# A delta-rule scan with two expert layers: the masked product of q and k with q's transposes narrowed first

## The chip, the cores and the metric

The kernel runs on one core of a Trainium2 chip. The metric is the device time of one launch in microseconds (us). Three runs of the kernel before took 901.98, 902.17 and 902.83 us, so the median is 902.17.

## The reference

Three parts follow each other; the change is in the first.

```python
# part 1: B, H, S, D = 4, 8, 768, 48
k_n = k / (norm(k) + 1e-6)
for t in range(S):
    y[t]  = q[t] @ state
    state = state + beta[t] * outer(k_n[t], v[t] - state.T @ k_n[t])
# part 2: x is y as (3072, 384)
h = x @ w_in; x = maximum(0.01 * h, h) @ w_out          # 2048 hidden
# part 3: 8 experts, routed per row
do = (x @ w_skip) > 0; e = argmax(x @ w_gate)
out = x + do * p[e] * (maximum(x @ w1[e], 0) @ w2[e])
```

## The kernel before

**Number form.** Nearly every matmul operand is held as two float16 parts, HI and LO. A product is three matmuls (HI·HI, LO·HI, HI·LO), the list `PARTS`. The HI part is a copy by ScalarE (`*_high`, all at L954), the LO part a subtraction by GpSimd or VectorE.

**Part 1 in groups.** The 768 steps are cut into 12 groups g of 64 (C). There are 32 heads in all; two of them lie on the 128 partitions, so a group has 16 units u (NU), in four steps of four (PAIRS). The scan needs, for each unit, the 64x64 products of a group's keys with its keys (`gram_a`) and of its keys with its queries (`gram_p`), the second masked to the entries above the diagonal.

- `turn_k`, `turn_q` (SyncE's queue) transpose the keys and queries of a group by DMA into `kT` and `qT`. Both are 128x128 per unit with two diagonal 64x64 blocks; the rest is zero.
- `compact_k` copies kT's two diagonal blocks by DMA next to each other into `kTc`, which is 64 columns wide.
- `gram_a(g, st)` is 12 matmuls of 64 columns (kT against kTc) into one PSUM bank.
- `gram_p(g, st)` is 12 matmuls of 128 columns (kT against qT). VectorE's `gram_p` (L1371) multiplies the bank with a mask into the float32 buffer `pm[st % 2]`, ScalarE's `p_high` (L954, operands<-masked) makes the HI half of `pT`, and GpSimd's `p_low` (L1898) the LO half. There are two `pm` buffers, so the third product waits for the first `p_low`.

**Order of the work.** Each engine's program is written out by hand. The main loop is `turn(g)` with 16 steps f. In every step TensorE does one `up` (9 matmuls of 256 columns, L743) and one `down` (6 of 384, L756) of part 2, for the rows of the group before. Between them stand the pieces of the scan of group g (steps 0 to 5, `scan_z` to `scan_s`, L682), `gram_a` of group g + 2 (steps 6 to 9) and `gram_p` of group g + 1 (steps 10 to 13).

One step's part 2 goes round the engines: `up` on TensorE, Relu on ScalarE (L1074), `leaky` on VectorE (L1483), the HI half on ScalarE (`hidden_high`, L954 stage<-stage), the LO half on GpSimd (`hidden_low`, L1908), `down` two steps later. `up` waits for the `leaky` two steps before.

VectorE also inverts a triangular system of group g + 1 in 33 small links (`inverse`, L1395 to L1415) which are dealt out over the steps by the table `SHARE`; its links L1398 and L1401 come in step 1. In step 0 and 1 it makes the z products for the scan (`scan_z` L1430, `scan_z_low` L1435), for which TensorE's `scan_u` waits.

Of the kernel before, what the change touches and what calls it, by code (L numbers as in the profile page):

```python
# [14 lines left out]
P = 128  # L15
# [4 lines left out]
def build(nc, q, k, v, beta, w_in, w_out, w_skip, w_gate, w1, w2, out):  # L20
# [39 lines left out]
    with ctx:  # L60
# [46 lines left out]

        kc = sb("kc", [P, 2 * NU * C], F16)
        kTc = kc[:].rearrange("p (l u i) -> p l u i", l=2, u=NU)
        ga = sb("ga", [P, NU, C])  # L110
# [121 lines left out]
        kc_copied = sem("kc_copied")  # L232
        kc_loaded = sem("kc_loaded")
# [184 lines left out]
        def _(sp):  # L418
# [16 lines left out]
            def turn_k(g):  # L435
                sp.wait_ge(kn_ready, 2 * g + 2)
                if g == 2:
                    sp.wait_ge(gp_done, B)
# [6 lines left out]
            def compact_k(g):  # L445
                sp.wait_ge(k_turned[g % 2], 32 * (g // 2) + 32)
                sp.wait_ge(ga_done, B * g)
                for x in range(2):
# [189 lines left out]
        def _(pe):  # L638
            def gram(rhs, g, st):
                n = rhs.shape[3]  # L640
                for p in range(PAIRS):
                    u = st * PAIRS + p
                    for a, b in PARTS:
                        mm = pe.matmul(b_gram[st % 2][:, p * n:(p + 1) * n], kT[g % 2][:, a, u, :], rhs[:, b, u, :],  # L644
                                       start=(p == 0 and (a, b) == PARTS[0]), stop=True, skip_group_check=True)
                return mm

            def gram_a(g, st):
# [13 lines left out]
                elif g:  # L662
                    pe.wait_ge(pm_ready, B * (g - 2) + 3)
                gram(kTc, g, st).then_inc(ga_done, 1)

            def gram_p(g, st):
                pe.wait_ge(q_turned, 32 * g + 32)
                if st >= 2:
                    pe.wait_ge(pm_ready, B * g + st - 1)
                elif is_group(g + 1):  # L670
                    pe.wait_ge(ga_ready, B * (g + 1) + st + 3)
                elif st == 1:
# [3 lines left out]
                gram(qT, g, st).then_inc(gp_done, 1)  # L676
# [10 lines left out]
            def scan_z(g, r):  # L687
                if r == 0:
                    pe.wait_ge(tr_free, tr_at["g", g - 2, 1] if g >= 2 else tr_at["x", 0, 1])
                else:  # L690
                    pe.wait_ge(pm_ready, B * g + B)
# [3 lines left out]
            def scan_u(g, r):  # L695
                pe.wait_ge(t_loaded, 128 * g + 128)
                pe.wait_ge(z_ready, 2 * g + r + 1)
                if g == 0 and r == 1:
                    pe.wait_ge(pm_ready, B)
# [73 lines left out]
            def gate_s(g, w):  # L773
                pe.wait_ge(tr_free, tr_at["g", g, w])
                if w == 0 and is_group(g + 2):
                    pe.wait_ge(pm_ready, B * (g + 2) + 3)
# [13 lines left out]
            def ranks(n):  # L790
                t0, t1 = BATCH[n]
                pe.wait_ge(hot_ready, n + 1)
                if n == 0:
                    pe.wait_ge(pm_ready, B * G)
# [85 lines left out]
            def turn(g):  # L880
                scan, nxt, ahead, gate = is_group(g), is_group(g + 1), is_group(g + 2), is_group(g - 1) and g < G
                scans = (scan_z, scan_u, scan_z2, scan_u2, scan_y, scan_s)
                for f in range(FT):
# [4 lines left out]
                    if nxt and f == 12:  # L888
                        gram_p(g + 1, 2 if g else 1)
# [8 lines left out]
                    if nxt and f in ((10, 11, 13) if g else (11, 13, 14)):  # L898
                        gram_p(g + 1, f - (10 if g else 11))
# [52 lines left out]
        def _(act):  # L952
# [36 lines left out]
            def p_high(g, st):  # L989
                act.wait_ge(pm_ready, B * g + st + 1)  # L990
                if g:
                    act.wait_ge(y_done, 2 * g)
                copy(units(pT, HI, st), pm[st % 2][:]).then_inc(p_hi, 1)
# [152 lines left out]
            def turn(g):  # L1146
                scan, nxt, ahead = is_group(g), is_group(g + 1), is_group(g + 2)
                gate, third = is_group(g - 1), is_group(g + 3)
                for f in range(FT):
# [12 lines left out]
                    if nxt and 12 <= f < (15 if g else 16):  # L1162
                        p_high(g + 1, f - (11 if g else 12))
                    if up_at(g, f):
                        hidden(*up_at(g, f))
                    if nxt and f == 11 and g:
                        p_high(g + 1, 0)
# [76 lines left out]
            for st in range(2):  # L1244
                p_high(0, st)
            for x in range(2):
                kn_high(2, x)
            for st in range(2, B):
                p_high(0, st)
# [83 lines left out]
        def _(dve):  # L1333
# [33 lines left out]
            def gram_p(g, st):  # L1367
                if B * g + st >= 2:
                    dve.wait_ge(p_ready, B * g + st - 1)
                dve.wait_ge(gp_done, B * g + st + 1)  # L1370
                dve.tensor_tensor(pm[st % 2][:], b_gram[st % 2][:], mask_p[:], ALU.mult).then_inc(pm_ready, 1)  # L1371
# [710 lines left out]
```

## Time and profile before

One execution was profiled; it took 900.34 us in all, and its span (first to last instruction) is 898.6 us.

| Engine | busy us | share of the span |
|---|---|---|
| TensorE matmuls | 776.0 | 86% |
| VectorE | 662.2 | 74% |
| ScalarE | 496.4 | 55% |
| GpSimd | 414.3 | 46% |

Part 1 with part 2 takes the first 690 us or so; the experts take the rest. Full turns are near 47 us long: step 10 of the turn shown below began at 499.48 us, the one before at 452.23 and the one behind at 545.58. In that region TensorE hardly stands still. A busy share of TensorE is not its speed: the matmuls overlap, and a group's true cost is read from the start of one group to the start of the next. VectorE's, ScalarE's and GpSimd's rows are durations as they were, waiting inside an instruction included.

### The profile page before, as it was taken

The page shows a single profiled execution, that of the slowest core. Times are in us where ns is not written, and L with a number is a line of the kernel's source. Part 1 is how long each engine was busy: PE and PEld are TensorE (multiplying, and loading weights), DVE is VectorE, ACT ScalarE, POOL GpSimd, SP SyncE. Part 2 cuts the span into 40 slices and gives each one's busy share as a digit, 9 for nine tenths or more (in the row PEclk, how much of TensorE's full clock was granted, in tenths as well). Part 3 has the DMA queues.
Part 4 walks back from the last instruction along what each step waited for, and adds up shares of the span by engine and source line. Part 5 has one row for each costly group of instructions (what it writes and reads, how often), then busy time and mean ns, then how long its engine had stood idle before and what let it go on. Part 6 is the DMA issues. An engine that isn't in the chain of part 4 may idle for free.

```text
span 898.6 us, 27698 instructions
## 1 busy us (share of the span) xinstructions
PE 776.0 (86%) x10782; PEld 625.4 (70%) x10783; DVE 662.2 (74%) x1334; ACT 496.4 (55%) x1108; POOL 414.3 (46%) x498
## 2 busy tenths in 40 slices
PE   0122679999999999999999999999999899999996
PEld 0122558787778787777878788878777777778774
DVE  6655978888887988887888887876768873563382
ACT  5426456767666666667676756554455651441261
POOL 5104153636354544535362724352352665564463
PEclk9995589999999999999999999999999999999998
DMA  9599177687687686868667686347416765263100
GB/s 214 148 233 163 28 116 123 133 140 143 116 149 133 120 162 113 133 124 138 127 121 149 114 144 121 77 71 231 169 30 200 246 230 188 70 214 120 44 16 16
DMA packets 357277, 119.76 MB, mean 133 GB/s; under 512 B 330450, under 2 KB 348420, under 8 KB 356784
## 3 DMA queue, kind: packets, MB, share of 16 engines
q1 hardware_dynamic: 351424, 104.33, 55.7%
q0 software_dynamic: 3232, 7.64, 2.5%
q10 hardware_dynamic: 2512, 6.29, 2.0%
q8 instruction: 73, 1.20, 0.5%
q14 instruction: 36, 0.29, 0.1%
HBM read 63.53 MB, written 21.25 MB: 94 GB/s over the span
## 4 chain that ended last, share of the span: by engine, by line
PE 37%; DVE 20%; issue 10%; SPq 10%; DMA 8%; ACT 8%; POOL 5%; DVEq 0%; POOLq 0%; ACTq 0%
PE b_h L743 8%; PE b_acc L756 8%; PE b_acc L849 7%; PE b_h L836 6%; DVE stage L1483 3%; PE b_ch L682 3%; SPq L442 2%; DVE inv L1409 2%; SPq L498 2%; ACT operands L954 2%; DMA operands<-operands 2%; SPq L510 2%; DVE inv L1415 2%; DMA operands<-nq 1%; PE b_gr L644 1%
## 5 line engine op out<-in xcount | busy, mean ns | idle before, releaser
L1908 POOL TENSOR_TENSOR stage<-stage 128x256 f16<-128x256 f32 x192 | 143.4, 747 | 246.9 <-ACT stage L954 246.0
L743 PE MATMUL b_h<-stage,wt 128*128 128x256 f16 x1728 | 221.8, 274 | 6.7 <-DVE stage L1342 6.3
L756 PE MATMUL b_acc<-wt,stage 128*128 128x384 f16 x1152 | 218.4, 326 | 3.7 <-POOL stage L1908 2.8
L743 PEld LDWEIGHTS b_h<-stage,wt 128*128 128x128 f16 x1728 | 159.1, 98 | 27.3 <-DVE stage L1342 8.2
L756 PEld LDWEIGHTS b_acc<-wt,stage 128*128 128x128 f16 x1152 | 106.7, 97 | 58.2 <-POOL stage L1908 5.7
L954 ACT ACTIVATE stage<-stage 128x256 f16<-128x256 f32 x192 | 80.0, 417 | 108.7 <-DVE stage L1483 107.8
L1483 DVE SCALAR_TENSOR_TENSOR stage<-b_h,stage 128x256 f32<-128x256 f32 x192 | 80.7, 420 | 42.1 <-ACT stage L1074 40.4
L849 PE MATMUL b_acc<-wt,operands 128*128 128x384 f16 x552 | 98.9, 330 | 7.1 <-DVE operands L1523 7.1
L836 PEld LDWEIGHTS b_h<-y,wt 128*128 128x128 f16 x1656 | 93.5, 98 | 6.5 <-issue 4.6
L836 PE MATMUL b_h<-y,wt 128*128 128x128 f16 x1656 | 96.5, 219 | 1.5 <-DVE y L1342 0.7
L1415 DVE TENSOR_REDUCE inv<-inv 128x30 f32<-128x90 f32 (+4 forms) x180 | 84.9, 472 | 5.6
L1074 ACT ACTIVATE stage<-b_h 128x256 f32<-128x256 f32 x192 | 72.1, 375 | 20.7 <-PE b_h L743 20.6
L849 PEld LDWEIGHTS b_acc<-wt,operands 128*128 128x128 f16 x552 | 52.7, 98 | 40.2 <-DVE operands L1523 8.7
L1898 POOL TENSOR_TENSOR operands<-masked,operands 128x512 f16<-128x512 f32 x48 | 56.9, 1187 | 43.6 <-ACT operands L954 43.4
L1409 DVE TENSOR_TENSOR inv<-a_sys,inv 128x60 f32<-128x60 f32 (+4 forms) x180 | 72.3, 402 | 1.8
L1144 ACT ACTIVATE operands<-b_h 128x512 f16<-128x512 f32 x48 | 28.6, 595 | 76.5 <-PE b_h L836 74.2
L682 PE MATMUL b_ch<-u,operands 128*128 128x48 f16 x1728 | 56.8, 185 | 11.5 <-DVE u L1440 8.8
L682 PEld LDWEIGHTS b_ch<-u,operands 128*128 128x128 f16 x1728 | 53.8, 97 | 15.3 <-issue 9.1
L1342 DVE SCALAR_TENSOR_TENSOR wt<-operands,wt 128x1536 f16<-128x1536 f32 (+1 forms) x36 | 58.3, 1623 | 4.1 <-ACT wt L954 3.9
L1523 DVE SCALAR_TENSOR_TENSOR operands<-b_h,operands 128x512 f16<-128x512 f32 x48 | 32.9, 687 | 31.7 <-ACT operands L1144 31.6
L2038 POOL DMA_INDIRECT out_dram<-y,id_out x24 | 29.6, 1235 | 57.3 <-issue 54.1
L644 PE MATMUL b_gr<-kc,operands 128*128 128x64 f16 x288 | 13.8, 203 | 47.5 <-DMA kc<-operands 30.6
(215 smaller groups left out, 1293.3 us busy)
## 6 DMA issues: line engine op xcount, KB each, us to landing
operands<-in_moe_w_dram SPq DMA_DIRECT2D x18, 1536.0 KB, 7.9
a_sys<-a_dram SPq DMA_DIRECT2D x24, 256.0 KB, 4.4
kc<-operands SPq DMA_DIRECT2D x22, 256.0 KB, 4.3
natq<-in_q_dram SPq DMA_DIRECT2D x24, 192.0 KB, 4.1
raw_v<-in_v_dram SPq DMA_DIRECT2D x24, 192.0 KB, 4.2
stage<-y SPq DMA_DIRECT2D x96, 48.0 KB, 2.0
x_dram<-stage SPq DMA_DIRECT2D x24, 192.0 KB, 2.8
out_dram<-stage SPq DMA_DIRECT2D x24, 192.0 KB, 3.4
```

The costliest lines, as they stand in the source:

```text
L682: mm = pe.matmul(b_ch[r][:, i * D:(i + 1) * D], lhs[:, a, u, :], rhs[:, b, u * D:(u + 1) * D], start=(first and i == 0 and (a, b) == PARTS ...
L743: mm = pe.matmul(b_h[f % 2][:, 0:GT], wt[0][:, a, d * FF + f * P:d * FF + (f + 1) * P], xT[:, g % 2, b, d, :], start=(i == 0), stop=(i == ...
L756: mm = pe.matmul(b_acc[w][:, 0:DM], g16[:, f % 4, a, w * P:(w + 1) * P], wt[1][:, b, f * DM:(f + 1) * DM], start=(f == 0 and (a, b) == PAR ...
L836: mm = pe.matmul(b_h[half][:, f * P:(f + 1) * P], ew[i][:, a, d * F1 + fc:d * F1 + fc + P], xgT[:, b, d * P:(d + 1) * P], start=(f == 0 an ...
L849: mm = pe.matmul(b_acc[0][:, 0:DM], e16[:, half, a, f * P:(f + 1) * P], ew[i][:, b, w0:w0 + DM], start=(half == 0 and f == 0 and (a, b) == ...
L954: return act.activation(o, i, ACT.Copy, scale=scale)
L1074: act.activation(r32[:, f % 2, :], b_h[f % 2][:, 0:GT], ACT.Relu, scale=0.99).then_inc(h_relu, 1)
L1342: return dve.scalar_tensor_tensor(o, i, scale, hi, ALU.mult, ALU.subtract)
L1409: dve.tensor_tensor(inv[:, 1:3].rearrange("p k (r i) -> p k r i", i=BLK)[:, :, 0:rows, c:BLK], a[:, c - 2:c, c:BLK].unsqueeze(2).to_broadc ...
L1415: dve.tensor_reduce(t_next[:, 0:rows, c:BLK], planes.rearrange("p k (r i) -> p r i k", i=BLK)[:, 0:rows, c:BLK], AX.X, ALU.add).then_inc(t ...
L1483: dve.scalar_tensor_tensor(g32[:, f % 4, :], b_h[f % 2][:, 0:GT], 0.01, r32[:, f % 2, :], ALU.mult, ALU.add).then_inc(g_ready, 1)
L1908: pool.tensor_tensor(g16[:, f % 4, LO, :], g32[:, f % 4, :], g16[:, f % 4, HI, :], ALU.subtract).then_inc(g_lo, 1)
```

## The change

1. VectorE copies the two diagonal blocks of `qT` into the narrow buffer (`compact_q`, two copies of 64 partitions x 2048 float16), in step 11. The buffer is the same as `kTc`, so `compact_k` of a later group waits for `gram_p`.
2. `gram_p` uses it: matmuls of 64 columns, in two steps of eight units (24 matmuls each) in steps 12 and 13, between `up` and `down`.
3. VectorE makes two masked products per group where it made four.
4. ScalarE and GpSimd write `pT` in four pieces as before, each now 64 partitions x 8 units x 64 columns (one diagonal block each). `pT` is zeroed once at the start. ScalarE's pieces move from steps 11 to 14 to steps 12 to 15, GpSimd's from 11 to 14 to 13, 14, 15 and 15.
5. GpSimd waits before each piece for its own last `hidden_low`, and behind each for the piece itself. Its constants for the routing (`constants`) move from steps 7 to 10 of turn 10 to steps 0 to 3 of turn 11.

```diff
+            def compact_q(g):
+                dve.wait_ge(q_turned, 32 * g + 32)
+                dve.wait_ge(ga_done, min(B * (g + 2), B * G))
+                for x in range(2):
+                    h = slice(C * x, C * x + C)
+                    dve.tensor_copy(qTc[h], qT[h, :, :, h]).then_inc(qc_copied, 1)
...
+            def gram_p(g, s):
+                pe.wait_ge(qc_copied, 2 * g + 2)
+                if is_group(g + 1):
+                    pe.wait_ge(ga_ready, B * (g + 1) + s + 3)
...
-                gram(qT, g, st).then_inc(gp_done, 1)
+                gram(b_gram[s], qTc, g, s * 2 * PAIRS, (s + 1) * 2 * PAIRS).then_inc(gp_done, 1)
...
-                    if nxt and f == 12:
-                        gram_p(g + 1, 2 if g else 1)
+                    if nxt and f in (12, 13):
+                        gram_p(g + 1, f - 12)
...
-                    if nxt and f in ((10, 11, 13) if g else (11, 13, 14)):
-                        gram_p(g + 1, f - (10 if g else 11))
...
+                h, u = slice(C * x, C * x + C), slice(s * 2 * PAIRS, (s + 1) * 2 * PAIRS)
+                copy(pT[h, HI, u, C * x:C * x + C], pm[s][h].rearrange("p (u c) -> p u c", c=C)).then_inc(p_hi, 1)
...
+                    if nxt and 13 <= f:
+                        p_high(g + 1, (f - 12) // 2, (f - 12) % 2)
...
+                    if nxt and f == 12:
+                        p_high(g + 1, 0, 0)
...
-                    if nxt and (11 if g else 12) <= f < (15 if g else 16):
-                        gram_p(g + 1, f - (11 if g else 12))
+                    if nxt and f == 11:
+                        compact_q(g + 1)
+                    if nxt and f in (12, 13):
+                        gram_p(g + 1, f - 12)
...
+            def p_low(g, s, x, before):
+                pool.wait_ge(p_hi, B * g + 2 * s + x + 1)
+                if before:
+                    pool.wait_ge(g_lo, FT * before[0] + before[1] + 1)
+                h, u, c = slice(C * x, C * x + C), slice(s * 2 * PAIRS, (s + 1) * 2 * PAIRS), slice(C * x, C * x + C)
+                pool.tensor_tensor(pT[h, LO, u, c], pm[s][h].rearrange("p (u c) -> p u c", c=C), pT[h, HI, u, c],
+                                   ALU.subtract).then_inc(p_ready, 1)
+                pool.wait_ge(p_ready, B * g + 2 * s + x + 1)
...
+                    if nxt and 13 <= f:
+                        p_low(g + 1, (f - 13) // 2, (f - 13) % 2, up_at(g, f - 1))
                     if up_at(g, f):
                         hidden_low(*up_at(g, f))
+                    if nxt and f == 15:
+                        p_low(g + 1, 1, 1, up_at(g, f))
```

VectorE around steps 11 to 14 of a turn, before: two of the four products and their neighbours.

```order
L1371 TENSOR_TENSOR masked<-b_gr,mask_p 128x512 [waits gp_done,p_ready]
L1409 TENSOR_TENSOR inv<-a_sys,inv 128x2x14x4 [waits t_link]
L1415 TENSOR_REDUCE inv<-inv 128x14x4 [waits t_link]
L1483 SCALAR_TENSOR_TENSOR stage<-b_h,stage 128x256 [waits g_lo,h_relu]
L1409 TENSOR_TENSOR inv<-a_sys,inv 128x2x15x2 [waits t_link]
L1415 TENSOR_REDUCE inv<-inv 128x15x2 [waits t_link]
L1371 TENSOR_TENSOR masked<-b_ch,mask_p 128x512 [waits gp_done,p_ready]
L1422 TENSOR_TENSOR inv<-inv 128x128x2 [waits t_hi]
L1422 TENSOR_TENSOR inv<-inv 128x128x2
L1483 SCALAR_TENSOR_TENSOR stage<-b_h,stage 128x256 [waits g_lo,h_relu]
L1371 TENSOR_TENSOR masked<-b_gr,mask_p 128x512 [waits gp_done,p_ready]
L1342 SCALAR_TENSOR_TENSOR stage<-b_tr,stage 128x384 [waits tr_hi]
```

The fourth product follows in step 14. In the changed kernel the same stretch of VectorE reads:

```order
L1377 COPY kc<-operands 64x2048 [waits ga_done,q_turned]
L1377 COPY kc<-operands 64x2048
L1421 TENSOR_TENSOR inv<-a_sys,inv 128x2x14x4 [waits t_link]
L1427 TENSOR_REDUCE inv<-inv 128x14x4 [waits t_link]
L1495 SCALAR_TENSOR_TENSOR stage<-b_h,stage 128x256 [waits g_lo,h_relu]
L1421 TENSOR_TENSOR inv<-a_sys,inv 128x2x15x2 [waits t_link]
L1427 TENSOR_REDUCE inv<-inv 128x15x2 [waits t_link]
L1383 TENSOR_TENSOR masked<-b_gr,mask_p 128x512 [waits gp_done,p_ready]
L1434 TENSOR_TENSOR inv<-inv 128x128x2 [waits t_hi]
L1434 TENSOR_TENSOR inv<-inv 128x128x2
L1495 SCALAR_TENSOR_TENSOR stage<-b_h,stage 128x256 [waits g_lo,h_relu]
L1383 TENSOR_TENSOR masked<-b_ch,mask_p 128x512 [waits gp_done,p_ready]
```

The copies stand ahead of two links of the inverse and of step 11's `leaky` (L1483 before, L1495 now), where one product stood; two products stand where three stood behind it.

GpSimd from the first LO piece on, before:

```order
L1908 TENSOR_TENSOR stage<-stage 128x256 [waits g_hi,kn_ready]
L1898 TENSOR_TENSOR operands<-masked,operands 128x512 [waits p_hi]
L1908 TENSOR_TENSOR stage<-stage 128x256 [waits g_hi]
L1898 TENSOR_TENSOR operands<-masked,operands 128x512 [waits p_hi]
L1908 TENSOR_TENSOR stage<-stage 128x256 [waits g_hi]
L1898 TENSOR_TENSOR operands<-masked,operands 128x512 [waits p_hi]
L1908 TENSOR_TENSOR stage<-stage 128x256 [waits g_hi]
L1898 TENSOR_TENSOR operands<-masked,operands 128x512 [waits p_hi]
L1908 TENSOR_TENSOR stage<-stage 128x256 [waits g_hi] x8
```

Behind the fourth piece comes a run of `hidden_low` without any. In the changed kernel the same stretch of GpSimd reads:

```order
L1928 TENSOR_TENSOR stage<-stage 128x256 [waits g_hi] x2
L1917 TENSOR_TENSOR operands<-masked,operands 64x8x64 [waits g_lo,p_hi]
L1928 TENSOR_TENSOR stage<-stage 128x256 [waits g_hi,p_ready]
L1917 TENSOR_TENSOR operands<-masked,operands 64x8x64 [waits g_lo,p_hi]
L1928 TENSOR_TENSOR stage<-stage 128x256 [waits g_hi,p_ready]
L1917 TENSOR_TENSOR operands<-masked,operands 64x8x64 [waits g_lo,p_hi]
L1928 TENSOR_TENSOR stage<-stage 128x256 [waits g_hi,p_ready]
L1917 TENSOR_TENSOR operands<-masked,operands 64x8x64 [waits g_lo,p_hi]
L1928 TENSOR_TENSOR stage<-stage 128x256 [waits g_hi,p_ready]
L1928 TENSOR_TENSOR stage<-stage 128x256 [waits g_hi] x5
```

The same four pieces now alternate with `hidden_low` one to two steps later: the last stands between the `hidden_low` of step 15 and that of step 0 of the next turn.

## Rows read from the trace of the kernel before

**Rows 1.** Busy time of each engine, one turn from step 10 to step 10.

```profile
core 0: us, PE busy (x) PEld busy (x) DVE busy (x) ACT busy (x) POOL busy (x), PEclk, DMA share, GB/s
499.48:545.58 46.10, 45.99 (x703) 37.83 (x703) 39.02 (x83) 31.12 (x80) 20.48 (x24) 1.00 0.72 132
```

**Rows 2.** TensorE's timeline, 491 to 525 us: start, length, instruction, idle before.

```profile
493.35 0.51 PE L644 MATMUL b_ch<-kc,operands 128*128 128x64 f16 x12
493.70 1.15 PE L743 MATMUL b_h<-stage,wt 128*128 128x256 f16 x9
...
501.45 0.83 PE L644 MATMUL b_gr<-operands 128*128 128x128 f16 x12
502.12 1.15 PE L743 MATMUL b_h<-stage,wt 128*128 128x256 f16 x9
...
505.73 0.83 PE L644 MATMUL b_gr<-operands 128*128 128x128 f16 x12
...
516.87 1.15 PE L756 MATMUL b_acc<-wt,stage 128*128 128x384 f16 x6
...
521.21 0.76 PE L682 MATMUL b_ch<-z,operands 128*128 128x48 f16 x24
```

**Rows 3.** Groups by line: one mask group; busy, mean ns, idle before, releaser.

```profile
L1371 DVE TENSOR_TENSOR masked<-b_gr,mask_p 128x512 f32<-128x512 f32 x24 | 16.2, 676 | 6.1 <-POOL operands L1898 6.1
```

**Rows 4.** Chain of waits, 18 to 24 us: start, length, what.

```profile
20.26 0.69 DVE kc L1736
...
20.98 2.03 DVE kc L1736
```

**Rows 5.** GpSimd's timeline at the same place.

```profile
20.33 2.12 POOL L1891 TENSOR_TENSOR operands<-natk,operands 64x768 f16<-64x768 f32 x1 [0.95 <-ACT operands L954]
```

**Rows 6.** VectorE's timeline, 491 to 525 us.

```profile
503.61 0.68 DVE L1371 TENSOR_TENSOR masked<-b_gr,mask_p 128x512 f32<-128x512 f32 x1
...
505.10 1.18 DVE L1409 TENSOR_TENSOR inv<-a_sys,inv 128x60 f32<-128x60 f32 x1
...
511.41 1.40 DVE L1342 SCALAR_TENSOR_TENSOR nq<-natq,nq 64x768 f16<-64x768 f32 x1
...
514.54 0.42 DVE L1483 SCALAR_TENSOR_TENSOR stage<-b_h,stage 128x256 f32<-128x256 f32 x1 [0.37 <-ACT stage L1074]
...
518.39 0.56 DVE L1435 TENSOR_TENSOR z<-scan,z 128x384 f16<-128x384 f32 x1
...
519.33 1.27 DVE L1398 TENSOR_TENSOR inv<-a_sys 128x512 f32<-128x512 f32 x1
520.52 0.54 DVE L1435 TENSOR_TENSOR z<-scan,z 128x384 f16<-128x384 f32 x1
```

**Rows 7.** GpSimd's timeline, 491 to 525 us.

```profile
503.58 0.67 POOL L1908 TENSOR_TENSOR stage<-stage 128x256 f16<-128x256 f32 x1 [0.54 <-ACT stage L954]
505.03 1.16 POOL L1898 TENSOR_TENSOR operands<-masked,operands 128x512 f16<-128x512 f32 x1 [0.78 <-ACT operands L954]
...
510.84 1.16 POOL L1898 TENSOR_TENSOR operands<-masked,operands 128x512 f16<-128x512 f32 x1 [0.96 <-ACT operands L954]
512.02 1.33 POOL L1908 TENSOR_TENSOR stage<-stage 128x256 f16<-128x256 f32 x1
...
515.49 1.33 POOL L1908 TENSOR_TENSOR stage<-stage 128x256 f16<-128x256 f32 x1
...
518.93 0.67 POOL L1908 TENSOR_TENSOR stage<-stage 128x256 f16<-128x256 f32 x1 [0.51 <-ACT stage L954]
```

**Rows 8.** ScalarE's timeline, 491 to 525 us.

```profile
513.61 0.63 ACT L954 ACTIVATE operands<-masked 128x512 f16<-128x512 f32 x1
...
516.27 0.36 ACT L1074 ACTIVATE stage<-b_h 128x256 f32<-128x256 f32 x1
```

**Rows 9.** Waits over the whole trace: total us, times, longest.

```profile
PE b_ch L682 <- DMA operands<-t_dram: 5.9, 4, 3.9
...
PE b_gr L644 <- DMA operands<-nq: 4.9, 3, 3.3
```

More of the change, by code:

```diff
@@ L638, in _, with gram @@
         def _(pe):
[L639 to L642, printed above, removed]
+            def gram(bank, rhs, g, u0, u1):
+                for u in range(u0, u1):
                     for a, b in PARTS:
-                        mm = pe.matmul(b_gram[st % 2][:, p * n:(p + 1) * n], kT[g % 2][:, a, u, :], rhs[:, b, u, :],
-                                       start=(p == 0 and (a, b) == PARTS[0]), stop=True, skip_group_check=True)
+                        mm = pe.matmul(bank[:, (u - u0) * C:(u - u0 + 1) * C], kT[g % 2][:, a, u, :], rhs[:, b, u, :],
+                                       start=(u == u0 and (a, b) == PARTS[0]), stop=True, skip_group_check=True)
                 return mm
@@ L1243, in _ @@
             root(2)
-            for st in range(2):
-                p_high(0, st)
+            for x in range(2):
+                p_high(0, 0, x)
             for x in range(2):
                 kn_high(2, x)
-            for st in range(2, B):
-                p_high(0, st)
+            for x in range(2):
+                p_high(0, 1, x)
             split_w_out(0)
@@ L1751, in _ @@
             dve.wait_ge(beta_ready, 1)
-            for st in range(B):
-                gram_p(0, st)
+            compact_q(0)
+            for s in range(2):
+                gram_p(0, s)
             split_w_out(0)
@@ L1919, in turn @@
                         s_low(g, f - 6)
[L1920 to L1921 removed]
+                    if nxt and 13 <= f:
+                        p_low(g + 1, (f - 13) // 2, (f - 13) % 2, up_at(g, f - 1))
                     if up_at(g, f):
                         hidden_low(*up_at(g, f))
[L1924 to L1925 removed]
+                    if nxt and f == 15:
+                        p_low(g + 1, 1, 1, up_at(g, f))
+                    if g == G - 1 and f < 4:
+                        constants(f)
                     if (g, f) == (G, 3):
@@ L1988, in _ @@
             tri(before16[:], 0, -1, 1, P, ALU.is_gt, 0.0)
-            m = mask_p[:].rearrange("p (u c) -> p u c", c=P)
-            link(pool.affine_select(out=m, in_=m, pattern=[[0, PAIRS], [1, P]], compare_op=ALU.is_gt, fill=0.0,
-                                    base=0, channel_multiplier=-1))
-            m = mask_p[0:C, :].rearrange("p (u c) -> p u c", c=P)[:, :, C:P]
-            link(pool.memset(m, 0.0))
+            for h in range(2):
+                m = mask_p[C * h:C * h + C].rearrange("p (u c) -> p u c", c=C)
+                link(pool.affine_select(out=m, in_=m, pattern=[[0, 2 * PAIRS], [1, C]], compare_op=ALU.is_gt, fill=0.0,
+                                        base=0, channel_multiplier=-1))
             for h in range(2):
@@ L2009, in _ @@
             pool.sem_inc(const_pool, 1)
+            link(pool.memset(pT.bitcast(F32), 0.0))
+            pool.sem_inc(const_pool, 1)
             pool.dma_start(spare_dram, row_id[:]).then_inc(yo_scattered, 16)
@@ L2013, in _ @@
                 kn_low(2, x, None)
-            for st in range(B):
-                p_low(0, st)
+            for s in range(2):
+                for x in range(2):
+                    p_low(0, s, x, None)
             for g in range(0, G + 1):
```

69 lines of the change are left out of this document (30 added, 39 removed).

## The prediction

> **What bounds the kernel now.** I looked first at a full turn by engine: of the 46.10 us from step 10 to step 10, TensorE's matmuls cover 45.99 and VectorE is busy for 39.02 [rows 1]. Then TensorE's timeline: the pieces follow each other without a gap, and only where another engine is late does the start move. So a turn is TensorE's, and whatever shortens TensorE's work is worth its full length unless the other engines' chain becomes late. That chain must be read from VectorE's and GpSimd's timelines side by side, because they hinder each other. VectorE's little link at 505.10 took 1.18 us and ended at 506.28, just behind GpSimd's instruction of 505.03 to 506.19; the copy of 0.69 us in the prologue took 2.03 when a GpSimd instruction stood in its way [rows 4 to 7]. It goes the other way too: `hidden_low` takes 0.67 us, but 1.33 at 512.02, where VectorE's product of 511.41 was at work until 512.81, after it had itself waited for the GpSimd piece that ended at 512.00 [rows 6, 7]. They take turns, a whole instruction each.
>
> The sums below are shifts, made on the profiled execution (900.34 us, span 898.6). It lies 1.83 us below the median of the three runs; I add the shifts to the median, 902.17.
>
> **TensorE's saving.** Twelve matmuls of 128 columns cost from 501.45 to 502.12, 0.67 us; twelve of 64 columns from 493.35 to 493.70, 0.35 [rows 2]. A group has four of these: 2.68 us before, 1.40 now, so 1.28 less. Over the eleven turns that hold one that is 14.1 us, the most this edit can bring there.
>
> The row for 64 columns bears on a rule. The Trainium skill ("TensorE: Matmul & The Clock Gate", section "LDWEIGHTS (loading the stationary operand)") puts a load of weights at columns / 1.2 ns, about 107 ns for 128 columns whatever the moving side; if that spaced the matmuls, 64 columns would cost as much as 128 and the saving would be 0 instead of 1.28 per group. By that rule the trace disagrees: 0.35 / 12 is 29 ns a pair [rows 2].
>
> **VectorE's two copies against two products.** A product costs 0.68 (mean 0.676) [rows 3, 6]. Removed: 1.36 us. The copy has its own rows in the prologue, in the same shape: 0.69 us free, and 2.03 where a GpSimd instruction (20.33 to 22.45) was in the way, which it outlived by 0.56 [rows 4, 5]. So a pair costs 1.38 to 2.72. In the turn, the product at 503.61 marks where the pair begins, and there `hidden_low` has just begun at 503.58 and holds until 504.25 [rows 6, 7]. One copy ends 0.56 later, at 504.81, the other 0.69 behind it, at 505.5. I take 1.9 us.
>
> What waits for it: TensorE's Gram in step 12 stands between `up` and `down`. Before, `up` of step 12 was through at 505.73 [rows 2]; without the two Grams of steps 10 and 11 (1.34) it is through at 504.39, and waits 1.1 us for the copies. Of 1.28 saved, 0.2 is left when step 13 is through. Behind the copies on VectorE stand two links and `leaky` of step 11, for which `up` of step 13 waits. They come 1.2 us later than now, but the link that cost 1.18 loses its GpSimd opponent (about -0.9), since no LO piece is in step 11 any more. `up` of step 13 begins near 507.5, after that `leaky`, so TensorE doesn't wait there. If the copies ran clear, this term would be 0.5 better.
>
> **Steps 13 to 15.** Here three of the four old LO pieces ran against VectorE's q halves: 511.41 took 1.40 and `hidden_low` 1.33, twice [rows 6, 7]. The pieces come later now, and by my placing both q halves start with GpSimd free. Without that, `leaky` of step 14 comes between 0.3 earlier and 0.1 later than 514.54, and the `hidden_low` that released TensorE's `down` at 516.87 (515.49 + 1.33 = 516.82) [rows 2, 7] ends between 516.1 and 516.8. TensorE may be up to 0.4 earlier here. Where copies of ScalarE are moved one step back their number is the same (four, 0.63 each [rows 8]); the last now stands ahead of the Relu of step 15, at 516.27, and with up to 0.3 gained before it, this Relu comes about 0.25 late.
>
> **Step 0 and 1 of the next turn, the new place of the fourth LO piece.** Now one `hidden_low` runs at 518.93 to 519.60, and VectorE's link L1398, begun at 519.33, ends at 520.60: 1.00 after the release [rows 6, 7]. Then z_low runs from 520.52 to 521.06, and TensorE's `scan_u` starts at 521.21, on its heels [rows 2, 6]. So this chain has no room: what is added to it is added to the turn. In the changed kernel a piece of 1.16 us [rows 7] comes between the `hidden_low` of step 15 (over near 518.6) and that of step 0. It starts at 518.7 if it gets in ahead of VectorE's product of 518.39, else behind it at 519.1 to 519.2 [rows 6], and ends between 519.9 and 520.3. L1398 then ends between 520.9 and 521.3, that is +0.3 to +0.7. The next `hidden_low` (0.67) is by then waiting too. As the GpSimd instruction slipped in between the two copies of the prologue [rows 4, 5], it can slip in between L1398 and z_low: +1.0 to +1.4. The ends for a turn, taken at `scan_u`, are therefore -0.4 (no collision, gain kept) and +1.4. Everything before is contained in these, because TensorE waits here for VectorE. I take 0.9, nearer to the collisions, which have rows, than to their absence.
>
> The Trainium skill ("SBUF — State Buffer", section "SBUF: two separate sides") says that VectorE and GpSimd share one port pair as an exclusive lock which a VectorE instruction takes when it has two SBUF inputs or runs in a two-port mode. That speaks against this change: a masked product reads PSUM and is free of it, a copy from SBUF to SBUF is not. The trace agrees in every pair above.
>
> **Where TensorE waited for transfers.** It waited 4.9 us in 3 times for q's transposes and 5.9 in 4 for the inverse (3.9 of it once, in the prologue) [rows 9]. So 6.9 us lie in about five turns. The Gram of q comes two steps later now, which takes most of its wait away; the other wait covers a late z_low. In five turns I count +0.3 instead of +0.9.
>
> **Prologue and the rest.** VectorE's wait of 6.1 us for GpSimd [rows 3] goes, since both products have a buffer of their own, but copies (1.4 to 2.7), 24 matmuls and the products stand ahead of ScalarE's key halves, and the LO pieces then run against VectorE's weight splitting. Taken as 0, ends -1 and +2. The first turn is bound by VectorE, which gets a wait for q's transposes: inside its +0.3 and this margin. GpSimd's extra waits for itself have each its own idle time ahead (it works 20.48 of 46.10 us [rows 1]). The constants of the routing move between two turns: 0. The later `compact_k` wait is met two turns ahead: 0.
>
> **Sum.** Six turns at +0.9 are 5.4, five at +0.3 are 1.5: +6.9. 902.17 + 6.9 = 909.1; I say 909.0.
>
> **Rivals.**
> - *The collisions add up everywhere.* All eleven turns at +1.3 and the first parts +1: 902.2 + 15.3 = 917.5. For it: turns repeat to within 0.1 us in their rows. Against it: the turns with a transfer wait have cover.
> - *Gain and loss cancel.* The fourth piece gets in early and `hidden_low` doesn't slip between: +0.3 less the waits given back, near 0 in all: 902.
> - *TensorE keeps part of it, the change is faster.* Place: the fourth LO piece misses L1398. If z_low is released by 520.7, `scan_u` can start up to 0.4 earlier: 11 x 0.4 = 4.4, 897.8. It decides at a z_low before 521.0. For it: TensorE does have less to do. Against: `hidden_low` of step 15 can't end before ScalarE's late Relu.
> - *All of it.* 902.2 - 14.1 = 888.1. It would need the copies to be done by 504.39, which would be 0.8 us from their start, less than the two take with no opponent.
>
> **Chances.** Forecast (903.98 to 914) 0.50; collisions everywhere 0.15; cancelled 0.15; part of the gain 0.16; all of it 0.04. The three runs before spread by 0.1%, so 0.2% (1.8 us) is what can be told from no change. Faster by more 0.20, within it 0.15, slower 0.65. The range leaves out the last case and the far end of the second: 898 to 916. The forecast's own range is 904 to 914.
>
> **What the new profile would show.** TensorE idle once a turn at step 12, about 1.1 us, released by the copies, and Grams of 24 matmuls 0.70 us apart; the first copy near 1.2 us and the second 0.69. L1410 (the old L1398) longer than 1.27 us, near 1.8, and a TensorE gap before `scan_u` of 0.7 to 1.6, released by z_low. The q halves near 0.95 instead of 1.40, `hidden_low` seldom at 1.33. I am wrong if the gap at `scan_u` is missing (then the time is below 903), or if the copies take 0.69 each or run at a slower rate without an opponent.

## The result and the profile after

| | before | after |
|---|---|---|
| median, same chip, 4 runs each | 902.08 us (900.58 to 902.83) | 913.01 us (912.67 to 915.8) |
| profiled span | 898.6 us | 910.9 us |
| TensorE, VectorE, GpSimd busy share, after | | 83%, 73%, 46% |

The changed kernel is slower: ratio 1.0136, 95% interval 1.0116 to 1.0157. The collisions and the wait that the prediction named were there; most terms of the turn had their size, and the start, the HI piece ahead of step 15's Relu and the sum over a turn were larger than forecast.

Where the time went is seen from the step in which TensorE first transposes y (step 7). Turn 1 reached it at 158.19 us before and at 161.83 after, so the prologue and turn 0 cost +3.6. The seven turns from there take 47.83 us each before and 48.95 after, +1.12. The rest adds 0.8 more; together that is the 12.3 by which the span grew.

TensorE's timeline after, in the same turn (group 8; its step 10 begins at 510.97, before at 499.48, so 11.49 is taken off to compare), answers to [rows 2]:

```profile
517.06 0.87 PE L648 MATMUL b_gr<-kc,operands 128*128 128x64 f16 x24 [1.02 <-DVE kc L1377]
517.77 1.14 PE L758 MATMUL b_acc<-wt,stage 128*128 128x384 f16 x6
...
526.79 1.16 PE L745 MATMUL b_h<-stage,wt 128*128 128x256 f16 x9 [0.22 <-DVE stage L1495]
...
531.52 0.76 PE L684 MATMUL b_ch<-z,operands 128*128 128x48 f16 x24 [0.41 <-DMA operands<-t_dram]
...
534.48 0.76 PE L684 MATMUL b_ch<-z,operands 128*128 128x48 f16 x24 [1.22 <-DVE z L1447]
```

The Gram of 24 matmuls takes 0.71 and waits 1.02 for the copies; `scan_u` of the second half waits 1.22 for z_low, and comes 1.78 later than before (521.21). VectorE there, against [rows 6]:

```profile
515.09 1.91 DVE L1377 COPY kc<-operands 64x2048 f16<-64x2048 f16 x2
...
517.60 0.41 DVE L1495 SCALAR_TENSOR_TENSOR stage<-b_h,stage 128x256 f32<-128x256 f32 x1
517.94 0.21 DVE L1421 TENSOR_TENSOR inv<-a_sys,inv 128x60 f32<-128x60 f32 x1
...
523.44 0.94 DVE L1347 SCALAR_TENSOR_TENSOR nq<-natq,nq 64x768 f16<-64x768 f32 x1
...
529.22 0.42 DVE L1495 SCALAR_TENSOR_TENSOR stage<-b_h,stage 128x256 f32<-128x256 f32 x1 [0.71 <-ACT stage L1079]
...
531.75 1.62 DVE L1410 TENSOR_TENSOR inv<-a_sys 128x512 f32<-128x512 f32 x1
533.30 1.03 DVE L1447 TENSOR_TENSOR z<-scan,z 128x384 f16<-128x384 f32 x1
```

GpSimd, against [rows 7]. The fourth LO piece (531.05) ran against L1410, and `hidden_low` (532.47), waiting by then, got its turn between L1410 and z_low; each of the two VectorE instructions paid for one:

```profile
530.24 0.67 POOL L1928 TENSOR_TENSOR stage<-stage 128x256 f16<-128x256 f32 x1 [0.69 <-ACT stage L954]
531.05 1.34 POOL L1917 TENSOR_TENSOR operands<-masked,operands 64x512 f16<-64x512 f32 x1
532.47 1.45 POOL L1928 TENSOR_TENSOR stage<-stage 128x256 f16<-128x256 f32 x1
```

ScalarE, against [rows 8]: the fourth HI piece stands between the inverse's seed and the Relu of step 15.

```profile
527.09 1.04 ACT L954 ACTIVATE inv<-eye_t 128x1024 f32<-128x1024 f16 x1
528.15 0.63 ACT L954 ACTIVATE operands<-masked 64x512 f16<-64x512 f32 x1
528.80 0.38 ACT L1079 ACTIVATE stage<-b_h 128x256 f32<-128x256 f32 x1
```

**The ring.** What orders these numbers is the interval from one `leaky` (L1483 before, L1495 after) to the next. `leaky` needs the Relu of ScalarE, that needs `up` of TensorE, and `up` needs a bank that an earlier `leaky` has freed. Before, `leaky` of steps 10 to 13 and 15 (step 14's is in [rows 6]):

```profile
502.56 0.42 DVE L1483 SCALAR_TENSOR_TENSOR stage<-b_h,stage 128x256 f32<-128x256 f32 x1 [0.58 <-ACT stage L1074]
504.77 0.41 DVE L1483 SCALAR_TENSOR_TENSOR stage<-b_h,stage 128x256 f32<-128x256 f32 x1
508.26 0.42 DVE L1483 SCALAR_TENSOR_TENSOR stage<-b_h,stage 128x256 f32<-128x256 f32 x1
511.06 0.42 DVE L1483 SCALAR_TENSOR_TENSOR stage<-b_h,stage 128x256 f32<-128x256 f32 x1 [0.23 <-ACT stage L1074]
...
516.81 0.41 DVE L1483 SCALAR_TENSOR_TENSOR stage<-b_h,stage 128x256 f32<-128x256 f32 x1
```

After, steps 10, 12, 13 and 14 (11 and 15 are above):

```profile
514.04 0.42 DVE L1495 SCALAR_TENSOR_TENSOR stage<-b_h,stage 128x256 f32<-128x256 f32 x1 [0.58 <-ACT stage L1079]
...
520.03 0.42 DVE L1495 SCALAR_TENSOR_TENSOR stage<-b_h,stage 128x256 f32<-128x256 f32 x1
523.10 0.43 DVE L1495 SCALAR_TENSOR_TENSOR stage<-b_h,stage 128x256 f32<-128x256 f32 x1 [0.50 <-ACT stage L1079]
526.30 0.42 DVE L1495 SCALAR_TENSOR_TENSOR stage<-b_h,stage 128x256 f32<-128x256 f32 x1 [0.36 <-ACT stage L1079]
```

In us, group 8's turn, with the last stretch from `leaky` of step 15 to the second `scan_u`:

| | 10-11 | 11-12 | 12-13 | 13-14 | 14-15 | to `scan_u` | sum |
|---|---|---|---|---|---|---|---|
| before | 2.21 | 3.49 | 2.80 | 3.48 | 2.27 | 4.40 | 18.65 |
| after | 3.56 | 2.43 | 3.07 | 3.20 | 2.92 | 5.26 | 20.44 |

The first stretch: two copies (1.91, of which 0.53 is the wait for the `hidden_low` of 515.06) stand where one product of 0.68 stood, which is 1.23 of the +1.35. The link that had cost 1.18 [rows 6] costs 0.21: most of -1.06. The HI piece before the Relu of step 15: +0.65. The fourth LO piece: +0.86. Together with +0.27 and -0.28 that is the +1.79 seen at `scan_u`. The changed kernel shows these intervals within 0.1 in each of turns 1 to 9. Before, the stretch 13-14 went from 3.47 to 4.81 and the last from 4.39 to 5.34 over the same turns.

### The profile page after: what moved, and what is told of

It reads as the page before. It is cut to its first block, busy times and chain, and to the rows that moved or that the text cites. A ratio compares the mean times of both kernels' runs of the same rounds, so it can differ in the third digit from the quotient of the medians.

```text
span 910.9 us, 27735 instructions
## 1 busy us (share of the span) xinstructions
PE 760.1 (83%) x10782; PEld 607.1 (67%) x10783; DVE 664.8 (73%) x1334; ACT 500.3 (55%) x1108; POOL 420.8 (46%) x499
## 4 chain that ended last, share of the span: by engine, by line
DVE 29%; PE 26%; ACT 17%; issue 14%; DMA 5%; SPq 4%; POOL 4%; ACTq 0%; DVEq 0%; POOLq 0%
PE b_acc L851 7%; DVE stage L1495 6%; PE b_h L838 6%; PE b_h L745 4%; PE b_acc L758 4%; ACT operands L954 4%; ACT stage L1079 3%; PE b_ch L684 3%; ACT stage L954 2%; DVE inv L1421 2%; ACT ga L954 2%; DVE kc L1377 2%; DVE inv L1427 2%; DVE z L1447 2%; ACT inv L954 2%
## 5 line engine op out<-in xcount | busy, mean ns | idle before, releaser
L745 PEld LDWEIGHTS b_h<-stage,wt 128*128 128x128 f16 x1728 | 159.7, 98 | 36.1 <-DVE stage L1347 8.7
L1495 DVE SCALAR_TENSOR_TENSOR stage<-b_h,stage 128x256 f32<-128x256 f32 x192 | 80.8, 421 | 49.8 <-ACT stage L1079 48.6
L648 PE MATMUL b_gr<-kc,operands 128*128 128x64 f16 x576 | 25.1, 201 | 71.3 <-DMA kc<-operands 30.9
L648 PEld LDWEIGHTS b_gr<-kc,operands 128*128 128x128 f16 x576 | 22.5, 103 | 76.4 <-issue 48.0
L1421 DVE TENSOR_TENSOR inv<-a_sys,inv 128x60 f32<-128x60 f32 (+4 forms) x180 | 65.1, 362 | 2.2
L1917 POOL TENSOR_TENSOR operands<-masked,operands 64x512 f16<-64x512 f32 x48 | 61.1, 1274 | 6.5
```

The lines of the kernel that those rows point to most:

```text
L745: mm = pe.matmul(b_h[f % 2][:, 0:GT], wt[0][:, a, d * FF + f * P:d * FF + (f + 1) * P], xT[:, g % 2, b, d, :], start=(i == 0), stop=(i == ...
L1421: dve.tensor_tensor(inv[:, 1:3].rearrange("p k (r i) -> p k r i", i=BLK)[:, :, 0:rows, c:BLK], a[:, c - 2:c, c:BLK].unsqueeze(2).to_broadc ...
L1495: dve.scalar_tensor_tensor(g32[:, f % 4, :], b_h[f % 2][:, 0:GT], 0.01, r32[:, f % 2, :], ALU.mult, ALU.add).then_inc(g_ready, 1)
L1917: pool.tensor_tensor(pT[h, LO, u, c], pm[s][h].rearrange("p (u c) -> p u c", c=C), pT[h, HI, u, c], ALU.subtract).then_inc(p_ready, 1)
```

## Experiments

Two theories stood at the start. *Collisions*: the change loses by VectorE and GpSimd in each other's way, at the copies and at the fourth LO piece; TensorE's saving is real and would come back. *Ring*: VectorE and ScalarE set the turn, TensorE's gapless rows only keep pace, so its saving is worth little. Results first (gaps: TensorE's idle time between 160 and 600 us; "turn": mean of seven turns; "start": when turn 1 reached step 7):

| run | start | turn | gaps | ratio to before, 95% |
|---|---|---|---|---|
| before | 158.2 | 47.83 | 9.7 | |
| after | 161.8 | 48.95 | 30.2 | 1.0136 (1.0116 to 1.0157) |
| e1 fourth LO piece out | 160.8 | 48.11 | 22.9 | 1.0067 (1.0041 to 1.0093) |
| e2 fourth LO piece late | 161.2 | 48.21 | 23.4 | 1.0059 (1.0039 to 1.0078) |
| e3 half the copy | 160.7 | 48.38 | 25.4 | 1.0087 (1.0056 to 1.0119) |
| e4 narrow Gram alone | 157.8 | 47.55 | 11.3 | 0.9981 (0.9966 to 0.9996) |
| e5 copy by DMA, late | 158.8 | 49.66 | 31.3 | 1.0187 (1.0123 to 1.0252) |
| e6 copies apart, late | 163.6 | 48.23 | 25.4 | 1.0079 (1.0056 to 1.0102) |
| e7 copies alone | 164.3 | 49.06 | 13.5 | 1.0193 (1.0141 to 1.0245) |
| e8 copy by DMA | 159.7 | 50.05 | 36.1 | 1.0207 (1.0153 to 1.0262) |
| e9 apart, a step earlier | 163.1 | 48.31 | 24.2 | 1.0093 (1.0069 to 1.0117) |
| e10 the same, first two by DMA | 160.2 | 48.14 | 22.0 | 1.0042 (1.0015 to 1.0069) |
| e11 both in step 10 | 159.5 | 48.50 | 26.8 | 1.0112 (1.0083 to 1.0141) |
| e12 Gram behind `down` | 158.6 | 48.24 | 19.5 | 1.0040 (1.0025 to 1.0056) |

**e1: the fourth LO piece left out** (its share of the product's low half is not computed).

```
-                    if nxt and f == 15:
-                        p_low(g + 1, 1, 1, up_at(g, f))
+                    if nxt and f == 15:
+                        pool.wait_ge(p_hi, B * (g + 1) + 4)
+                        pool.sem_inc(p_ready, 1)
```

> The changed kernel with the fourth LO piece of q's masked product left out (GpSimd only signals it; the LO half of eight units' second head stays zero or old). Theory (the loss is the collision of that piece with VectorE's link and z product in steps 0 and 1): TensorE's gap before scan_u, 1.22 us a turn, falls to 0.3 or less; ten turns give back about 1.2 each, so 901 us, between 899 and 904. Rival (the loss is made in steps 11 and 12 by the two copies): the turn keeps its length, 911 to 913.

Measured 907.21 against 900.92 of before. The stretch to `scan_u` is 4.40 again; the others stay at 3.56, 2.43, 3.06, 3.21, 2.92. So the collision is real, and worth half the loss; the other half stands elsewhere. The time lies between what the two theories said.

**e2: the fourth LO piece in step 2 of the next turn**, all work done.

```
-                    if nxt and f == 15:
-                        p_low(g + 1, 1, 1, up_at(g, f))
+                    if scan and g and f == 2:
+                        p_low(g, 1, 1, up_at(g, f))
```

> The changed kernel with the fourth LO piece made in step 2 of the next turn, behind that step's hidden_low, where GpSimd stands idle for over 1 us. All work is done. Theory: as without the piece, 900 to 905, unless it meets VectorE there too (z and u products of steps 2 and 3), which would leave up to 0.5 a turn: then 906. Rival (copies): 911 to 913.

906.23: as e1. The piece costs by its place, not by its work.

**e3: only the HI half of q's transposes is copied** (the LO half of the narrow copy keeps old values).

```
-                    dve.tensor_copy(qTc[h], qT[h, :, :, h])
+                    dve.tensor_copy(qTc[h, HI], qT[h, HI, :, h])
```

> The changed kernel with only the HI half of q's transposes copied (the copies are half as long, 0.36 instead of 0.69; the LO half that the Gram reads is an old one). Theory (collision): TensorE's gap in step 12 shrinks from 1.02 to about 0.4, but scan_u still waits for VectorE, so the turn gets shorter by 0 to 0.3: 910 to 913. Rival (copies are the cause): 0.65 a turn in eleven turns, 906.

908.86, again between the two expectations. The ring's first stretch falls from 3.56 to 3.02, the rest stays.

**e4: the kernel before, two of three matmuls of q's Gram 64 columns wide**, no copy (LO terms of the second half of the columns are left out).

```
+                        m = n if (a, b) == PARTS[0] else C
-                        ... rhs[:, b, u, :]
+                        ... rhs[:, b, u, 0:m]
```

> The kernel before with its Gram of q as it was, but two of the three matmuls of each unit cut to 64 of the 128 columns, without any copy (the second head of each unit gets no correction terms). It saves TensorE 8 x 4 x 27 ns = 0.85 us a turn and adds nothing. Theory (the z product's chain in steps 0 and 1 has no room, so TensorE's time is worth little): 0 to 0.3 a turn, 899 to 902. Rival (a turn is TensorE's, as its 45.99 busy of 46.10 say): 0.85 x 11 = 9.4, 893.

```profile
499.05 0.62 PE L645 MATMUL b_gr<-operands 128*128 128x128 f16 x12
499.51 1.15 PE L744 MATMUL b_h<-stage,wt 128*128 128x256 f16 x9
```

(The row gives the form of the first of its matmuls.) 898.91 against 900.92. TensorE has 0.85 less to do in a turn (four Grams at 0.46 instead of 0.67) and the turn is 0.28 shorter; in group 8's, the ring reads 2.21, 3.50, 2.80, 3.32, 2.27, 4.40: the same as before but for 0.16. This speaks for the ring: before the change TensorE showed hardly a gap (9.7 us in 440), and still most of what it was spared didn't come back. The column of gaps hides this, since the matmuls' rows overlap. From start to start, with every group of matmuls at the shortest spacing that it repeats, TensorE's work from step 7 of turn 8 to step 7 of turn 9 is 45.5 of 46.9 us before and 44.7 of 46.8 in e4: of the 0.85 saved, 0.14 shortened this turn and 0.71 became standing time.

**e5 and e8: the narrow copy made by DMA** (e5 with the fourth piece late as well), issued by SyncE behind `load_q`.

```
+            def compact_q(g):
+                sp.wait_ge(q_turned, 32 * g + 32)
+                sp.wait_ge(ga_done, min(B * (g + 2), B * G))
+                for x in range(2):
+                    h = slice(C * x, C * x + C)
+                    sp.dma_start(qTc[h].rearrange("p l u i -> p (l u) i"),
+                                 qT[h, :, :, h].rearrange("p l u i -> p (l u) i")).then_inc(qc_copied, 16)
```

> The changed kernel with two edits: q's narrow copy is made by two DMAs from q's transposes (issued by SyncE after the key Gram of step 9), not by VectorE; and the fourth LO piece runs in step 2 of the next turn. All work is done. Both edits together take every suspected VectorE/GpSimd collision out of the turn. Collision theory (what was lost is the copies on VectorE plus the fourth piece): the gap at step 12 (8.1 us in nine turns before) and the one at z_low (2.3) go, TensorE's gaps between 160 and 600 us fall from 23.4 to about 13, and the time falls from 906.2 to 897 to 900, a little faster than the kernel before. Rival, the chain theory (another chain of ScalarE and VectorE work sets the turn as soon as TensorE is shorter): the gaps move to other places, and the time stays above 902. Second rival, the transfer comes late: a DMA of such a copy takes 4 us to land, so TensorE waits for it at step 12, 0.5 to 1.5 us a turn, and in turn 0, where it stands behind q's transposing, 2 to 4 us: 902 to 910.

> The changed kernel with q's narrow copy made by two DMAs, not by VectorE; the fourth LO piece stays where the change put it, between the two hidden_low of steps 15 and 0. All work is done. It completes a table of two by two (copies by VectorE or by DMA; fourth piece early or late). If the two losses add: 913 - (906.2 - the time with both edits), so 904 to 907. If they don't (a loss at z_low is covered by one at step 12): the gap at z_low stays near 11 us in nine turns and the time is within 2 us of 913.

917.66 and 922.50 against 902.65: my theory fell. Of the rivals, the first only said that the gaps would move and the time stay above 902; the second named TensorE's wait for the copies, which came (8.1 us in e5 and 13.4 in e8 between 160 and 600 us), but it is the smaller part in e5. In e5 the ring is short (2.10, 2.44, 3.06, 3.46, 2.91), so VectorE is freed as hoped, but the inverse's transfer comes late. TensorE in e5:

```profile
518.13 0.87 PE L659 MATMUL b_gr<-kc,operands 128*128 128x64 f16 x24 [0.18 <-DMA kc<-operands]
534.60 0.78 PE L695 MATMUL b_ch<-z,operands 128*128 128x48 f16 x24 [2.79 <-DMA operands<-t_dram]
```

The wait for t_dram is 17.7 us in nine turns (3.6 after). The DMA list of e5 shows 24 copies more and a longer time from issue to landing for the store of the inverse:

```profile
kc<-operands SPq DMA_DIRECT2D x46, 256.0 KB, 4.2
...
t_dram<-inv SPq DMA_DIRECT2D x24, 128.0 KB, 3.5
```

In the changed kernel these are x22 and 2.6 us; in the kernel before the store took 3.0. How the copies slow the inverse is not shown. In group 8's turn of e5 they had landed 5.21 us after TensorE's step 10, before the store was issued (8.42); the store landed at 13.89 (13.65 in e2), and the last of the eight loads of the inverse at 21.68 (20.74 in e2), just when TensorE's wait ended. The two losses do not add: late placing saves 0.8% beside VectorE's copies, and 0.2% with intervals that overlap beside the DMAs.

**e6: copies apart, behind `leaky` of steps 10 and 11**, fourth piece late.

```
-                    if nxt and f == 11:
-                        compact_q(g + 1)
+                    if nxt and g and f in (10, 11):
+                        compact_q(g + 1, f - 10, f - 9)
```

> The changed kernel with the fourth LO piece in step 2 of the next turn, and VectorE's two copies apart: from turn 1 on the first stands in step 10 and the second in step 11, each behind leaky, where VectorE waited 0.6 us for ScalarE. All work is done. The second copy should end near 515.8 on the changed kernel's time axis instead of 517.0, when TensorE is ready at 516.0. Theory that the place of the copies matters: the gaps at step 12 fall from 8.1 us to under 2 and the time from 906.2 to 899 to 901. Rival, the copies' work matters wherever they stand (VectorE is 1.9 us a turn fuller against 1.36 taken off): the inverse's links and the later steps come late instead, the gap moves to the wait for the inverse or for leaky, and the time stays at 904 to 907.

910.26. I had the place wrong: `leaky` of step 11 starts 5.4 us after TensorE's step 10, so the second copy ended later than before, and TensorE waited 1.52. Each copy ran alone, at 0.68 and 0.69, and yet the ring's first two stretches (2.33 and 3.62) add up to the 5.98 of e2 within 0.03: keeping the copies clear of GpSimd gave nothing at this place.

**e7: the kernel before with the copies added**, unused, in ten turns and the prologue.

```
+                    if nxt and g < G - 2 and f == 11:
+                        compact_q(g + 1)
```

> The kernel before with only the two copies added to VectorE, in step 11 ahead of its first masked product of q; nothing uses them, they go into the narrow copy's buffer. Ten of the eleven turns and the prologue have them. What stays as before: four wide Grams, four products of 512 columns, LO pieces in steps 12 to 15. The copies take 1.9 to 2.7 us a turn here, as a LO piece... and hidden_low stand against them. Theory that VectorE has little room in these steps: the masked products, leaky and hidden_low of steps 11 to 13 come late by 1 to 1.5 us, and the time rises by 10 x 0.8 to 10 x 1.3: 909 to 915. Rival (VectorE works 39 of 46 us, so the copies go into its idle time): 901 to 904.

```profile
518.11 1.90 DVE L1375 COPY kc<-operands 64x2048 f16<-64x2048 f16 x2
```

919.37. The ring reads 4.15, 3.50, 2.81, 3.32, 2.27, 4.39: +1.94 in the first stretch, nothing in the others. TensorE hardly shows a gap (13.5 us in nine turns), since it has its old, longer Grams. The loss is +6.1 at the start, +8.6 in the seven turns (1.23 each) and +1.9 behind them. The expectation of 909 to 915 was short by the start.

**e9, e10, e11: other places.** e9 as e6 with the copies at the head of steps 10 and 11; e10 the same with DMAs for the first two groups; e11 with both copies at the head of step 10.

```
 e9, e10:  +   if nxt and g and f in (10, 11):
           +       compact_q(g + 1, f - 10, f - 9)
 e11:      +   if nxt and g and f == 10:
           +       compact_q(g + 1)
 e10, e11: +   if g < 2:
           +       pe.wait_ge(qc_loaded, 32 * g + 32)
```

> As the run with copies apart and the fourth LO piece late, but from turn 1 on the first copy stands at the start of step 10 and the second at the start of step 11, each a leaky earlier (about 2.3 to 3 us) than there. In that run TensorE was ready for its Gram 5.07 us after it began step 10, and the second copy ended 6.53 us after; now it should end at 5.1 to 5.5. All work is done. Theory that only the place of the copies is wrong: the gap at step 12 falls from 12.6 us to under 3 in nine turns, a turn from 48.2 to 47.4, and the time to 897 to 901. Rival, VectorE has no room whatever the place: leaky of step 10, the inverse's links or the wait for the inverse come late by as much, a turn stays at 48.0 to 48.3 us, and the time at 904 to 908.

> The run before this one with one more edit: for the first two groups (the prologue and turn 0) q's narrow copy is made by DMAs; VectorE makes it only from turn 1 on. All work is done. In the run where all copies were by DMA, turn 1 reached its step 7 at 158.8 us, against 161.2 to 161.8 where VectorE made them and 158.2 before. Theory that the prologue and turn 0 cost 3 us through these copies: 2 to 3 us below the run before, 894 to 898 if that one is at 897 to 901. Rival (the start's loss is of another kind, as the key halves that stand behind the LO pieces): within 1 us of the run before.

> The run before this one, but both copies stand together at the start of step 10. They end near 2 us after TensorE's start of step 10, 3 us before they are wanted; leaky of step 10, which had 0.6 us of idle time ahead, comes 0.8 us late. If only the wait at step 12 counts: same as the split within 1 us, with no gap at step 12 at all. If VectorE's leaky and the links bind: TensorE waits for leaky 0.5 us a turn or for the inverse, and the time is 3 to 6 us above the split.

911.80, 906.34 and 914.09 against 903.49. The waits for the copies shrink from 8.1 us (e2) to 3.7 in e9 and e10 and to none in e11, but others take their place: in e11 the wait for `leaky` (13.0 us against 1.8 in e2), in e9 and e10 more of it (3.9 and 2.9) and of the wait for the inverse's transfer (8.6 and 7.4 against 5.6). The sum of gaps stays at 22 to 27. The place did move the ring: its first stretch is 2.84 in most turns of e9 and e10 against 3.56, and their shortest turns take 47.3 us against 48.1 in e2; in the mean over seven turns the waits for transfers took this back. In group 8's turn of e11 VectorE first waits for q's transposes, then both copies stand against GpSimd's key piece:

```profile
506.61 3.25 DVE L1393 COPY kc<-operands 64x2048 f16<-64x2048 f16 x2 [0.32 <-DMA operands<-nq]
```

```profile
506.59 0.67 POOL L1943 TENSOR_TENSOR stage<-stage 128x256 f16<-128x256 f32 x1 [0.70 <-ACT stage L969]
507.41 1.90 POOL L1923 TENSOR_TENSOR operands<-natk,operands 64x768 f16<-64x768 f32 x1
```

e10 speaks for the copies at the start: 2.9 us less than e9 at step 7 of turn 1, and a ratio 0.5% lower. A single profile says this to some 2.4 us only: e2, e6 and e9 are the same program up to that step and reached it at 161.2, 163.6 and 163.1.

**e12: TensorE's first Gram behind `down`**, copies as in the change, fourth piece late, first two groups by DMA.

```
-                    if nxt and f in (12, 13):
-                        gram_p(g + 1, f - 12)
+                    if nxt and f == 13:
+                        gram_p(g + 1, 1)
                     if down_at(g, f):
                         down(*down_at(g, f))
+                    if nxt and f == 12:
+                        gram_p(g + 1, 0)
```

> The changed kernel, all work done, with three edits: the fourth LO piece late (step 2 of the next turn); q's narrow copy of the first two groups by DMAs, VectorE's two copies together in step 11 from turn 1 on, where the change has them; and TensorE's first Gram of q stands behind `down` of step 12, not ahead of it. The copies end 1.0 us after `up` of step 12 and `down` takes 0.97, so `down` fills the wait, the Gram starts where it did, and its product comes no later. Theory that the changed kernel loses by this wait because it stands in TensorE's order at that place: the gap at step 12 goes from 8 us to under 1 in nine turns, nothing else gets later, a turn falls from 48.1 to 47.3, and with the start's 3 us the ratio to before is 0.992 to 0.997. Rival (the ring of `up`, leaky, hidden and `down` through VectorE sets the turn: VectorE's copies and not TensorE's wait for them are the loss): the gap turns up at leaky, at `down`'s hidden or at the inverse, a turn stays at 47.8 to 48.1, and the ratio is 1.000 to 1.004.

906.04 against 902.16, ratio 1.0040. TensorE's wait for the copies is gone in every turn:

```profile
507.67 1.14 PE L773 MATMUL b_acc<-wt,stage 128*128 128x384 f16 x6
508.85 0.87 PE L660 MATMUL b_gr<-kc,operands 128*128 128x64 f16 x24
...
518.58 1.16 PE L760 MATMUL b_h<-stage,wt 128*128 128x256 f16 x9 [0.41 <-DVE stage L1512]
```

and the ring did not move: 3.55, 2.43, 3.07, 3.21, 2.91, 4.41, the same as e1 and e2 within 0.02. The rival was right: in this ring the 1.02 us at step 12 was no loss of its own, only the place where TensorE stood still. No version beat the kernel before; e4, which does, leaves work out.

## Why the prediction was right and where it was wrong

- *TensorE's saving, 1.28 a group.* The size is right (0.71 for 24 matmuls). Its worth was not: "whatever shortens TensorE's work is worth its full length unless the other engines' chain becomes late". That chain was already almost the limit; of 0.85 taken off, 0.28 a turn came back (e4). This is the step that failed at the root, though the forecast passed it on only as 0.2 at step 13. The profile had a hint: in the turn TensorE's matmuls are busy for 45.99 us of 46.10, its weight loads only for 37.83, less than VectorE's 39.02 [rows 1].
  The Trainium skill ("Perfetto Trace Analysis", section "Identifying the Most-Contended Engine") says that TensorE's matmul busy time is no good measure of how close it is to its limit and wants its rate of arithmetic and the busy share of weight loads instead; by the weight loads, VectorE is the most contended engine here. The runs agree: e4's saving on TensorE was worth a third, while e7's copies on VectorE (1.90) lengthened the ring's first stretch by 1.94 and a turn by 1.23 in the mean.
- *The copies.* Predicted 1.9 and a wait of 1.1; measured 1.91 and 1.02. Predicted for `leaky` of step 11 1.2 later, and 0.9 back from the link; measured 1.35 and 1.06. Right, and TensorE's wait was rightly seen but wrongly priced: it is a symptom (e12).
- *Steps 13 to 15.* The q halves took 0.94 and 0.96 (0.95 predicted). `leaky` of step 14 came 0.27 later, outside -0.3 to +0.1; it is the net of the first two stretches (1.35 - 1.06), the next two cancel. The HI piece ahead of the Relu of step 15 was mis-sized: the Relu came 1.04 late (528.80 less 11.49, against 516.27) instead of 0.25. The prediction set up to 0.3 of gain against the piece's 0.63; instead `up` of step 15 came 0.27 late.
- *Steps 0 and 1.* Both collisions came as described: L1410 took 1.62, and `hidden_low` slipped in ahead of z_low (1.03). The piece cost 0.86. But the bound of +1.4 for a turn was for a turn that arrives on time; this one came to step 15 with 0.93 already lost, and +1.78 resulted.
- *Transfer waits.* Against the even +0.3 the seven turns from step 10 of turn 1 to step 10 of turn 8 gave +1.66, +0.88, +1.03, +1.78, +0.17, +0.63 and +1.69. Cover by such waits exists, in two of seven rather than in five of eleven. The kernel before doesn't repeat as closely as the prediction says ("to within 0.1 us"): its seven intervals go from 47.14 to 48.80, those of the changed kernel from 48.93 to 48.97.
- *Prologue and first turn*, taken as 0 and +0.3, range to +2: +3.6. Turn 0 pays 2.7 of it. There the copies waited 1.09 for q's transposes and TensorE 3.69 for the copies, where before it waited 3.27 for the transposes themselves; afterwards it waited for `leaky` and `hidden_low`. Mis-sized, and the largest single miss. For the copies as its cause: start at 158.6 to 160.2 us in the five runs with DMAs there, 160.7 to 163.6 in those with VectorE's copies, 164.3 where they came on top. The groups stay apart, though runs of one program differ by up to 2.4 within them. A lower granted clock isn't the reason: from 90 to 110 us it was 0.50 in e2 and 1.00 in e6 and e9, which came later.
- *Sum.* +6.9 predicted, +10.9 by the medians. What follows step 7 of turn 1 gave 8.7 of span (6.6 predicted), the start 3.6 (0.3 predicted). 913.0 is 1 us inside the upper end of the range; that the start's miss still fitted is luck. The rival in which TensorE keeps part of its gain needed the piece to miss L1398 (now L1410); e2 made it miss, and no gain appeared.

## What to carry to other kernels

An engine without a gap need not be the bound: where it passes work round a ring of buffers with other engines, compare the ring's interval with the engine's own work, and test the saving alone (e4, one run) before paying for it. A wait that appears on one engine is not a price until taking it away shortens the ring (e12). Work moved to VectorE costs its time there and a turn of GpSimd's at each instruction that both can be at.

## What the hardware showed that I had not expected

- Two copies of 0.69 us took 3.25 against two GpSimd instructions (e11), 1.41 when free and 1.91 against one. The GpSimd side pays too: `hidden_low` 1.45 instead of 0.67. Whoever waits gets the next turn, even between two VectorE instructions that follow each other.
  The Trainium skill ("SBUF — State Buffer", section "SBUF: two separate sides") says that whichever starts first holds the shared ports for its whole instruction. The traces agree, and add who comes next.
- Half the partitions save nothing: 64x512 took GpSimd 1.15 us and ScalarE 0.63, as 128x512 had [rows 7, 8].
- Two DMAs of 256 KB a turn, which take no compute engine's time, cost more than VectorE's copies did: ratio 1.0187 (e5) against 1.0059 (e2), with TensorE waiting 17.7 us for the inverse's transfer against 5.6. How they delay it stays open.
